# Loads in another order, and the first batch's (states @ w1) copied on chip: a fused attention and two mixture-of-experts kernel in float32

## The reference

```python
def _attn_ref(x, state):
    scores = scale * x @ state^T;   a = softmax(scores);   xread = a @ state
    scores2 = scale * state @ x^T;  a2 = softmax(scores2); sread = a2 @ x
    return concatenate([xread, sread], axis=2)      # (B, H, S + Ns, D)

# the rows of all heads side by side: x of shape (2304, 512)
def _moe_ref(x, w_gate, w1, w2):                    # E = 8 experts, F = 1024
    P = exp(x @ w_gate - max), made doubly stochastic in 8 rounds
    for e in range(E):
        out += P[:, e:e + 1] * (relu(x @ w1[e]) @ w2[e])
def _moe2_ref(...):                                 # the same, but one expert per row
    out[mask] = gate * sigmoid(...) * (relu(x[mask] @ w1[e]) @ w2[e])
```

## Time and profile before

| | |
|---|---|
| median of 3 runs | 1620.22 us (1617.74 to 1624.94) |
| the profiled execution | 1622.05 us |
| its span in the profile | 1620.3 us, 20524 instructions |
| first load issued by SP | 0.82 us after the start of the span |
| first product on PE | 9.81 us |
| start of hidden(0) | 38.99 us |

### The profile page before, as it was taken

The page is one execution under the profiler, slowest core; times in us unless marked ns, Lnnn a source line. Parts: engine busy times, 40 slices in busy tenths (PEclk is TensorE's granted clock), DMA queues, the critical chain, the costliest instruction groups (busy, mean ns, idle before and its releaser), DMA issues.

```text
span 1620.3 us, 20524 instructions
## 1 busy us (share of the span) xinstructions
PE 1556.9 (96%) x7288; PEld 1258.0 (78%) x7289; DVE 632.5 (39%) x1010; ACT 516.3 (32%) x873; POOL 53.6 (3%) x73
## 2 busy tenths in 40 slices
PE   4899999999999999999999999999999996999997
PEld 3687868877877887788778877877888885888885
DVE  4545464334333523342333334333422226535221
ACT  4433343233223413331332234223312222435121
POOL 1000000000000000000000000000000001111110
PEclk9889999999999999999999999999999987999998
DMA  7530134134213412330332034112310233444110
GB/s 195 158 85 27 53 112 155 34 103 124 60 53 104 124 33 78 109 115 12 104 124 85 27 105 130 52 55 95 100 32 27 91 130 130 146 147 138 39 41 15
DMA packets 111908, 143.57 MB, mean 89 GB/s; under 512 B 33040, under 2 KB 65808, under 8 KB 111824
## 3 DMA queue, kind: packets, MB, share of 16 engines
q1 hardware_dynamic: 107104, 131.70, 25.8%
q0 software_dynamic: 3200, 9.70, 1.8%
q10 hardware_dynamic: 1520, 1.05, 0.2%
HBM read 99.93 MB, written 43.25 MB: 88 GB/s over the span
## 4 chain that ended last, share of the span: by engine, by line
PE 92%; DVE 3%; DMA 2%; ACT 1%; issue 1%; SPq 0%; ACTq 0%; POOL 0%; DVEq 0%; POOLq 0%
PE PS L834 15%; PE PS L835 14%; PE PS L836 14%; PE PS L820 7%; PE PS L822 7%; PE PS L821 7%; PE PS L600 3%; PE PS L982 2%; PE PS L1005 2%; PE PS L1007 2%; PE PS L983 2%; PE PS L984 2%; PE PS L1006 2%; PE PS L590 1%; PE PS L992 1%; PE PS L874 1%
## 5 line engine op out<-in xcount | busy, mean ns | idle before, releaser
L834 PE MATMUL PS<-w2h,hTh 128*128 128x512 f32 x1024 | 408.8, 399 | 0.0
L835 PE MATMUL PS<-w2l,hTh 128*128 128x512 f32 x1024 | 400.0, 391 | 0.0
L836 PE MATMUL PS<-w2h,hTl 128*128 128x512 f32 x1024 | 399.4, 390 | 0.0
L1460 DVE SCALAR_TENSOR_TENSOR hTl<-PS,hTh 128x512 fp32r<-128x512 f32 x256 | 177.0, 691 | 559.3 <-ACT hTh L1132 559.1
L1132 ACT ACTIVATE hTh<-PS 128x512 fp32r<-128x512 f32 x256 | 153.0, 598 | 672.0 <-PE PS L822 672.0
L834 PEld LDWEIGHTS PS<-w2h,hTh 128*128 128x128 f32 x1024 | 192.8, 188 | 61.9 <-DVE hTl L1460 18.9
L836 PEld LDWEIGHTS PS<-w2h,hTl 128*128 128x128 f32 x1024 | 192.6, 188 | 41.1
L835 PEld LDWEIGHTS PS<-w2l,hTh 128*128 128x128 f32 x1024 | 192.9, 188 | 37.2
L820 PE MATMUL PS<-aTh,swh 128*128 128x512 f32 x512 | 201.5, 394 | 9.2 <-DVE swl L1456 8.0
L822 PE MATMUL PS<-aTh,swl 128*128 128x512 f32 x512 | 199.8, 390 | 0.0
L821 PE MATMUL PS<-aTl,swh 128*128 128x512 f32 x512 | 199.8, 390 | 0.0
(11 more groups left out here) (225 smaller groups left out, 1586.2 us busy)
## 6 DMA issues: line engine op xcount, KB each, us to landing
sw_rows<-swout SPq DMA_DIRECT2D x128, 256.0 KB, 2.4
swraw<-sw_rows SPq DMA_DIRECT2D x512, 64.0 KB, 2.2
raw<-in_moe_w SPq DMA_DIRECT2D x10, 2048.0 KB
w1raw<-in_moe_w SPq DMA_DIRECT2D x69, 256.0 KB, 3.1
w2raw<-in_moe_w SPq DMA_DIRECT2D x64, 256.0 KB, 2.8
x_in<-in_x SPq DMA_DIRECT2D x16, 256.0 KB, 4.6
x_rows<-acc SPq DMA_DIRECT2D x16, 256.0 KB, 2.7
w1raw<-in_moe_w ACTq DMA_DIRECT2D x3, 256.0 KB, 6.9
```

The lines of the kernel that those rows point to most:

```text
L834: mm(PS[:, 4 + j, :], hTh[:, i % 2, ts], w2h[:, fc, :], start=(fc == 0), stop=False)
L835: mm(PS[:, 4 + j, :], hTh[:, i % 2, ts], w2l[:, fc, :], start=False, stop=False)
L836: last = mm(PS[:, 4 + j, :], hTl[:, i % 2, ts], w2h[:, fc, :], start=False, stop=(fc == CF - 1))
L1460: V.scalar_tensor_tensor(out=hTl[:, i % 2, :], in0=PS[:, 0, :], scalar=0.0, in1=hTh[:, i % 2, :].bitcast(F32), op0=ALU.max, op1=ALU.subtra ...
```

## The change

1. The states are loaded by two transfers of 256 KB that are first in SP's queue, side by side in `st_in` (u = 0, 1 hold the same), with no memset before them. Eight transposes take the place of 16. x of batch 0 is issued half by SP and half by ACT.
2. For batch 0 of expert 0 `direct_sw(k)` copies 32 rows of each sw block from SBUF to `swraw`. Only batches 1 to 3 (96 rows) of chunks 0 to 7 go to DRAM. Chunks 0 to 3 are kept in `first_out`, which lies where w2h will be; ACT waits for their eight stores (`sw_first`) before `high_w2(0)`.
3. `sw_rows` has another layout: [expert parity, half, batch, group, 128 rows, 512]. A load of a quarter is one transfer where it was four; a store's DRAM side is one block of 32 rows for each batch, where it was 128 rows without a gap.
4. SP's list has another order: x(1) comes behind the stores of chunks 0 to 3, x(2) and x(3) later, w1 chunks 8 to 10 at steps 5 to 7.
5. The first four w1 subtractions move from POOL to DVE. The lists of attention_first and of steps 0 to 17 are written anew on all three engines; x_turn(1) moves out of attention_first, its first part in front of hidden(1), and hidden(0) no longer waits for x(1).

```diff
-        sw_rows = nc.dram_tensor("sw_rows", [2, 2, CD, 2, B, NS, BANK], F32, kind="Internal").ap()
+        sw_rows = nc.dram_tensor("sw_rows", [2, 2, B, G, P, BANK], F32, kind="Internal").ap()
...
+            def direct_sw(k):
+
+                half, c = k // CD, k % CD
+                for u in range(2):
+                    g = 2 * k + u
+                    sp.wait_ge(sw_out[u], k + 1)
+                    src = first_out[0:NS, g, :] if half == 0 else swout[0:NS, g % OUT_RING, :]
+                    row = (c % 2 * 2 + u) * NS
+                    dst = swraw[row:row + NS, 2 * half:2 * half + 2, c // 2, :]
+                    ins = sp.dma_start(dst, src.rearrange("p (q f) -> p q f", q=2))
+                    ins.then_inc(sw_direct[half], 16)
+
             def store_sw(k):
 
                 e, half, c = chunk_of(k if k < 2 * CD else k + 2 * CD)
                 for u in range(2):
                     g = 2 * k + u
                     sp.wait_ge(sw_out[u], k + 1)
-                    dst = sw_rows[e % 2, half, c, u].rearrange("b r f -> (b r) f")
-                    sp.dma_start(dst, swout[:, g % OUT_RING, :]).then_inc(sw_stored[g % OUT_RING], 16)
+                    rows = slice((c % 2 * 2 + u) * NS, (c % 2 * 2 + u + 1) * NS)
+                    if k < CD:
+                        sp.dma_start(sw_rows[e % 2, half, 1:B, c // 2, rows, :], first_out[NS:P, g, :]).then_inc(sw_first, 16)
+                    elif k < 2 * CD:
+                        sp.dma_start(sw_rows[e % 2, half, 1:B, c // 2, rows, :],
+                                     swout[NS:P, g % OUT_RING, :]).then_inc(sw_stored[g % OUT_RING], 16)
+                    else:
+                        sp.dma_start(sw_rows[e % 2, half, :, c // 2, rows, :],
+                                     swout[:, g % OUT_RING, :]).then_inc(sw_stored[g % OUT_RING], 16)
...
+                src = sw_rows[e % 2, half, b, :, :, f0:f0 + 256].rearrange("g r f -> r g f")
+                sp.dma_start(swraw[:, q % SW_RING, :, :], src).then_inc(sw_loaded[q % SW_RING], 16)
+
+            for u in range(2):
+                sp.dma_start(st_in[:, :, u, :], state.rearrange("b (g r) n d -> (r n) (b g) d", r=4)).then_inc(state_loaded, 16)
+            load_x_rows(sp, 0, 0)
+            load_x_rows(sp, 0, 1)
+            load_w1(1)
+            load_w1(3)
+            load_w2(0)
+            direct_sw(0)
+            load_w1(4)
+            direct_sw(1)
+            direct_sw(2)
+            direct_sw(3)
+            load_w2(1)
+            load_w1(5)
+            for k in range(CD):
+                store_sw(k)
             load_x(1)
...
             load_w1(6)
             load_w1(7)
+            load_w2(2)
+            load_w2(3)
+            for k in (CD, CD + 1):
+                direct_sw(k)
+                store_sw(k)
...
@@ PE @@
             states_chunk(4, 2)
-            pe.wait_ge(xT_ready, 8)
             states_chunk(5, 6)
+            pe.wait_ge(x_loaded[1], 16 * J)
+            pe.wait_ge(sub_done, 2)
+            x_turn(1, 0, 1)
...
@@ ACT, attention_first @@
                 keep_sw(0, 0, 6)
+                exp_tokens(0)
+                keep_sw(1, 0, 2)
                 high_w1(2)
-                exp_states(0)
-                keep_sw(1, 0, 2)
                 high_w1(3)
-                exp_tokens(0)
...
                 high_sw(0)
+                high_w1(4)
+                exp_states(0)
                 high_w1(5)
+                act.wait_ge(sw_first, 16 * 2 * CD)
                 high_w2(0)
                 high_h(0)
                 keep_sw(4, 0, 2)
...
@@ DVE, attention_first @@
                 keep_sw(0, 7)
                 keep_sw(1, 3)
+                low_w1(2)
                 sum_tokens(0)
-                sum_states(0)
+                low_w1(3)
+                max_states(0)
```

More of the change, by code:

```diff
@@ L133, in attention_then_two_moes @@
         lgT, _ = place("lgT", [2 * E, N], F32, xT_at)
-        st_bd, _ = place("st_bd", [P, PAIRS, P], F32, h_at)
+        st_in, _ = place("st_in", [P, B * G, 2, DH], F32, h_at)
+        first_out, _ = place("first_out", [P, 2 * CD, BANK], F32, w2_at)
         a1, _ = place("a1", [P, J * H * NS], F32, sT_at)
@@ L231, in attention_then_two_moes @@
         sw_out = [sem(f"sw_out{u}") for u in range(2)]
+        sw_first, sw_direct = sem("sw_first"), [sem(f"sw_direct{half}") for half in range(2)]
         s_step, s_relu, sT_done, sT_hi, sT_lo = sem("s_step"), sem("s_relu"), sem("sT_done"), sem("sT_hi"), sem("sT_lo")
@@ L364, in load_sw @@
                 half = quarter // 2
-                stores = 4 * CD * e + (4 * CD if half else 2 * CD)
-                for s in range(OUT_RING):
-                    sp.wait_ge(sw_stored[s], 16 * (stores // OUT_RING))
+                if e == 0 and half == 0:
+                    sp.wait_ge(sw_first, 16 * 2 * CD)
+                else:
+                    stores = 4 * CD * (e - 1) + (4 * CD if half else 2 * CD) + 2 * CD
+                    for s in range(OUT_RING):
+                        sp.wait_ge(sw_stored[s], 16 * (stores // OUT_RING))
                 if q >= SW_RING:
@@ L398, in _ @@
                 if i < 2:
+                    direct_sw(CD + 2 + i)
                     store_sw(CD + 2 + i)
[L400 removed]
                 for m in chunks_at(i):
@@ L408, in _ @@
                 if i == 1:
-                    load_sw(2)
-                    load_sw(3)
-                if i and i % 2 == 0 and i // 2 + 3 < E * QUARTERS:
+                    load_x(2)
+                if i and i % 2 == 0 and 4 <= i // 2 + 3 < E * QUARTERS:
                     load_sw(i // 2 + 3)
@@ L635, in attention_first @@
                 pe.wait_ge(pool_made, MADE_FIRST)
-                pe.wait_ge(state_loaded, 16 * 4)
-                for q in range(PAIRS):
-                    last = tr(PS[:, 4 + q // 4, (q % 4) * P:(q % 4 + 1) * P], st_bd[:, q, :], ident[:, :])
+                pe.wait_ge(state_loaded, 16 * 2)
+                for k in range(B * G):
+                    last = tr(PS[:, 4 + k // 4, (k % 4) * P:(k % 4 + 1) * P],
+                              st_in[:, k, :, :].rearrange("p u d -> p (u d)"), ident[:, :])
                 last.then_inc(stT_done, 1)
@@ L690, in attention_beside @@
+                    states_weights_turn(0, 1, 3)
+                elif i == 3:
+                    pe.wait_ge(xT_ready, 8)
+                    states_scores(1, 0, 1)
+                    pe.wait_ge(a2T_ready, 1)
+                    states_scores(1, 1, 2)
+                    pe.wait_ge(a2T_ready, 2)
+                    pe.wait_ge(gates_loaded, 48)
+                    states_read(0, 3)
+                elif i == 4:
                     pe.wait_ge(s2_ready, 4)
                     scores_turn(1, 0, 1)
-                    pe.wait_ge(sw_out[0], 8)
@@ L720, in attention_beside @@
                     pe.wait_ge(sr_lo, 1)
                     pe.wait_ge(gws_lo, 1)
-                    x_turn(2, 2, 3)
-                elif i == 6:
+                    pe.wait_ge(x_loaded[2], 16 * J)
+                    x_turn(2, 0, 3)
+                elif i == 5:
+                    pe.wait_ge(sub_done, 3)
+                    x_turn(2, 1, 1)
+                    pe.wait_ge(sub_done, 4)
+                    x_turn(2, 2, 2)
+                    pe.wait_ge(xT_ready, 9)
+                    x_turn(2, 3, 3)
+                elif i == 6:
+                    pe.wait_ge(a1_ready, 2)
+                    pe.wait_ge(xT_ready, 10)
+                    weights_turn(1, 0, 1)
+                    pe.wait_ge(xT_ready, 11)
+                    weights_turn(1, 1, 2)
+                    pe.wait_ge(xT_ready, 12)
+                    pe.wait_ge(a2_ready, 2)
+                    states_weights_turn(1, 0, 3)
+                elif i == 7:
+                    pe.wait_ge(aT_lo, 3)
+                    states_weights_turn(1, 1, 1)
+                    pe.wait_ge(aT_lo, 4)
+                    states_scores(2, 0, 2)
@@ L724, in attention_beside @@
                     pe.wait_ge(a2T_ready, 3)
-                    x_turn(2, 3, 1)
+                    states_scores(2, 1, 3)
                     pe.wait_ge(a2T_ready, 4)
[L727 to L731, removed]
+                    states_read(1, 1)
                 elif i == 8:
                     pe.wait_ge(s2_ready, 6)
-                    scores_turn(2, 0, 1)
+                    scores_turn(2, 0, 2)
@@ L1047, in _ @@
             A = nc.scalar.activation
-            act.wait_ge(zeroed, 1)
-            for r in range(4):
-                dst = st_bd[r * NS:(r + 1) * NS, :, :].rearrange("n (k u) m -> n k u m", u=2)
-                src = state.rearrange("b (g r) n d -> r n (b g) d", r=4)[r]
-                act.dma_start(dst[:, :, r // 2, (r % 2) * DH:(r % 2 + 1) * DH], src).then_inc(state_loaded, 16)
-            for m in range(W1_RING):
+            load_x_rows(act, 0, 2)
+            load_x_rows(act, 0, 3)
+            for m in (0, 2):
                 e, half, c = chunk_of(m)
@@ L1174, in attention_first @@
```

(17 more changed lines are left out.)

330 lines of the change are left out of this document (140 added, 190 removed).

## The result

| | before | changed |
|---|---|---|
| median | 1621.48 us (4 runs) | 1677.11 us (1675.63 to 1677.95, 4 runs) |
| ratio | | 1.0337, 95% interval 1.0323 to 1.0351 |
| span of the profiled execution | 1620.3 us | 1675.1 us |

The changed kernel is 3.4% slower, some 56 us, and the time lies 41 us above the range that was forecast. The direction that was likeliest in the text (slower, at 47%) is right, the place of the first wait as well, and so is the reason for it, but the text put 5.4 us at the start and 2.9 behind it where the spans show about 15 and 40.

The account below looks back on a forecast made before the run. PE was taken as the bound, busy 1556.9 of 1620.3 us. To the profiled 1622.05, +5.4 up to output(7) and +2.9 at the handover gave 1630.3; less 1.8 for the median, 1628.5 us, range 1607 to 1636.

Parts of the forecast that it names:

- the first wait: After hidden(0) and chunks 4 and 5, PE idles from 38 us until x(1) lands at 58.4.
- 5.4 us at the start: Up to output(7): 4.9 us later, plus 0.5 for chunk 7's direct copy queued behind chunk 6's stores.
- States and x first: Start of the kernel: states count from 7.5 us, not 9.8; x's transposes end at 12.6, against 15.8.
- DVE as the bound: Before hidden(0): four subtractions add 2.8 us on DVE, spending the early lead; hidden(0) at 32.6, 6.4 us earlier.
- Three engines a store, and x(1) behind them: Eight first stores, 2.7 us each, take 21.5 us, through at 52.8; x(1) queued behind them lands at 58.4.
- From there to output(7): From x(1)'s landing to the end of output(7): 57.8 us, ending at 116.2 against 111.3.
- rival 2: Three engines, and PE idles before step 3 or 4, so states_read(0) is slow again: 1635 us; chance 15%.
- in steps of two they fit: Later experts: 16 stores of 2.7 us in some 150 us fit, crowding only where expert 0 hands over.
- the +2.9 us of the hand-over: Where expert 0 hands over, two w1 chunks come late behind stores: +2.9 us, from 0 to 5.
- Rival 1: All 16 engines carry the stores, x(1) lands at 40.9, output(7) ends 12.6 us earlier: 1608 us; chance 20%.
- the bound to "same": 1628.3 us, where a measurement tells 0.5% (8.1 us) from no change; slower got 47%, same 35%.

Follow-up runs that it names:

- e7: e1 with the first four w1 subtractions on POOL again, not DVE: 1609.95 us, ratio 0.995.
- e1: The changed kernel with the old layout of sw_rows (stores of one run of 96 or 128 rows, four loads a quarter): 1614.37 us, ratio 0.996.
- e2: The kernel before with only the new layout of sw_rows (stores of four blocks, one load a quarter): 1691.5 us, ratio 1.0437.
- e3: The changed kernel, layout and single loads kept, with each store issued block by block: 1621.28 us, ratio 0.9995.
- e4: The changed kernel with only the stores from expert 1 on issued block by block: 1640.26 us, ratio 1.0121.
- e9: e5 with the first stores issued between the direct copies, not behind the last: 1604.38 us, ratio 0.9889.
- e5: e1 with x(1) loaded before the first direct copy: 1609.62 us, ratio 0.9934.
- e8: e1 without the copies on chip; 128 rows are stored and all quarters loaded back: 1608.43 us, ratio 0.9928.
- e11: e8 with x(1) loaded early: 1609.07 us, ratio 0.9917.

## Why the prediction was wrong, by its steps

- **States and x first**: right. The states' transposes begin at 7.3 (7.5 forecast), and stTl's pair took 1.40 us where it took 2.5. x's transposes end at 14.4, later than the 12.6 of the text, but chunk 0 begins at 17.49, forecast 17.0.
- **DVE as the bound**: right. Chunk 3 starts at 28.38 (forecast 27.0, before 27.1), behind sum_tokens; e7 gives the 2 us back. hidden(0) at 34.70 for 32.6: chunk 3 began 1.4 us later than forecast and ran at the lower clock (0.50 from 28 to 31 us).
- **Three engines a store, and x(1) behind them**: right, and shown by e1, e2 and e3. The Trainium skill's rule (DMA: Bandwidth & Descriptors, "Why a DMA increments its semaphore by 16 and not by 1") gives just these engine counts. The runs agree: 25 GB/s for each of three or four blocks. PE is back at 62.34, forecast 58.4; 2.5 of the 3.9 us are the stores' later issue.
- **From there to output(7)**: 57.8 forecast, 65.2 measured (from 62.34 to 127.15 + 0.39). It is off by the wait of 5.26 for direct copy 7, behind six stores, and by the lower clock behind that wait: 1.5 us in hidden(4) and 1.6 in the scores. The text had the copy land at 78 with 0.5 us to pay; in the changed kernel it reached ACT at 85.8. So output(7) ends 16.3 us later than before (127.5 for 111.3; 15.2 by the tile copies, of which the one before began 1 us after its tile was ready), where +5.4 was forecast. The condition of rival 2 came true (PE idles in front of step 3), and a price of about its 2.8 us for the neighbours too; the low clock in states_read(0), which it was named for, did not.
- **The step that failed is the one that reads "in steps of two they fit", and the +2.9 us of the hand-over.** The queue does have room for 16 stores of 2.7 us in an expert. But the question was what each load behind them may lose, and the text put nothing on it. SP issues a quarter's load only when the store in front of it has its data. From issue to need there are 3.8 us (425.80 - 5.03 - 416.95). The old loads landed in 2.2; this one had two stores in front, which take some 5.2 (two times 64 KB at 25.3 GB/s), and landed in 8.8. e4 puts the term at 37 us, hand-over included, where 2.9 stood. In the hand-over it was 16 us and not 5. The text let the two stores in front of a w1 chunk begin on idle engines, and gave the chunk 6.0 us from issue to ACT (227.7 - 221.75); it took 10.3. From 235.7 to 236.4, before that pair was issued, the queues already moved 102 GB/s at a DMA share of 0.26, as with four engines, so the pair before was most likely still running. How the 16 us are shared between this and the late chunks pushing the next stores, no run separates.
- **The bounds** were therefore too narrow: the range took 5 us for everything behind step 7. Rival 1 (16 engines) was given 1608; e1, which makes it true, measures 1614.4: x(1)'s transposes begin at 48.17 and not at 40.9, as chunk 3 and the copies behind it came later and SP issued x(1) only at 40.76. That "slower" came out likeliest was close: the forecast lay on the bound to "same", and it was the term that the text had missed that made it clear.

## What to carry to other kernels

A new layout in DRAM changes how many DMA engines a store uses: keep many rows outermost on both sides (96 and 128 were fast here, 3 and 4 blocks slow), or cut the transfer so that it has them (32 rows here, at some 0.47 us of SP for each issue), and read GB/s and DMA share of the first such stretch. A transfer on few engines delays not only itself but all that is queued behind it, so its price is each follower's slack, counted from when its queue really issues it, not from where its line stands. In an in-order queue a wait put in for something urgent holds back what is ready; the copy on chip paid off only after both x(1) and the stores were moved out from behind it (e9 1604 us; e5, with x(1) alone moved, 1610, and e8 and e11, without the copy, 1608 and 1609).

## What the runs showed of the hardware

- The rate of one DMA engine in a 2 KB row store is about 25.4 GB/s, whether three or four run (76 and 102 GB/s); the weight loads, on all 16, reach 389, or 24.3 each.
- SP itself is held while few engines drain: eight issues took 13.95 us in the changed kernel and 5.39 in e1.
- The first scores (eight 128x512 products) took 1.94 us in the changed kernel and 3.68 in e1, with the same instructions in front; the granted clock from 15.5 to 19.5 us is 1.00 in both profiles. Seven of the other profiles of the rewritten lists are on e1's side, at 3.5 to 3.7, and e4 and e5 on the other. What makes it so was not tried. Hidden(0) came 2.3 us later in e1, so a single profile can't tell a change of that size.
